# The first batch's gate convolution on TensorE as products with diagonal matrices, and the opening loads and splits in another order

## The chip, the cores and the metric

The kernel runs on one core of one Trainium2 chip. The metric is the device time of one execution in microseconds (us), lower is better. The kernel before takes 1178.61 us, the median of three runs (1178.06 to 1179.55).

## What is computed

Three stages follow each other, for four batches of 576 positions (the reference, cut):

```python
scores = scale * np.matmul(q, k.transpose(0, 1, 3, 2))       # 4 x 8 heads, 576 x 576, 64 dims
kth = np.partition(scores, -32, axis=-1)[..., -32:-31]
attn = softmax(np.where(scores >= kth, scores, -1e9))
x = concat_heads(np.matmul(attn, v))                          # 4 x 576 x 512
gate_pre[:, s, :] = sum(conv_w[k] * xp[:, s + k, :] for k in range(5))   # xp: 4 zero rows, then x
x = sigmoid(gate_pre) * (x @ w_val) @ w_out
u = x + np.real(np.fft.fft(np.fft.fft(x, axis=1), axis=2))
out = u + np.maximum(norm(u) @ w_ch1, 0) @ w_ch2              # 512 -> 2048 -> 512
```

The convolution is per feature: each of the 512 features has its own five taps.

## The kernel before

Every engine has its own list of instructions, written out in one function for each engine (sync for the DMA queue, tensor, scalar, vector, gpsimd), and they meet by semaphores. All five run the same main loop over **slots**, `for s in plan`. A tile is 128 query rows of one head (or the last 64 rows of both heads of a pair); a pair of heads has 9 tiles (`TILES`), a batch 4 pairs, 36 tiles (`NT`). In slot s tile s enters and older tiles move on:

- TensorE, `scores(s)` (L442): fp32r products of the high parts of the queries with high and low parts of the keys. `transpose_p(s-6)` (L455) turns the exponents of tile s-6. `attend(s-7)` (L471, L475) multiplies with v where a unit of the output ends (tiles 1, 3, 5, 7 and 8 of a pair); it needs the reciprocal of the sums.
- ScalarE, in this order: `copy_scores(s)` (L648), `store_pT(s-6)` (L668), `exponent(s-5)` (L655, L660), `split_weights(s-2)` (L686), the step of the second half of the kernel, `store_out(s-7)` (L677), `gate_tanh` (L690), then the high parts for the next pair (`high_queries` L635 to L638, `high_keys` L642).
- VectorE: in odd slots `reciprocal(s-6)` (L801, L803), in even ones `select(s-1, 0)`, then for odd slots the rest of a pair of tiles, `select(s-2, 1)`: four MAX8 (L761, L776) and three MATCH_REPLACE8 (L770) for each tile, two tiles taken in turn, to find the 32nd value of each row. Then the low parts of the second head of the next pair (`split_low`, L790, L792), and `conv` (L816, L819): five taps of 128 x 576 for a channel chunk c of 128 features, one chunk for each pair of heads.
- POOL: `biases(s-5)` (L917, L918; needs the 32nd value), `split_weights(s-2)` (L934), `scale_out(s-7)` (L929, writes x_new, the input of the convolution), low parts of the first head of the next pair (`split_low`, L907, L909).

In slots 2 to 33 the 32 parts of w_ch1 and w_ch2 are split into a high (fp32r) part by ScalarE and the rest by POOL, and written back to DRAM for the later passes. They come through two buffers, u[0] and u[1].

Four feature matrices' products (`feature_weights`, L482) run in slots 6, 8, 10 and 12. From slot 43 on, the steps of the batch before (values L482, the Fourier products, projection, and the two layers of 2048, L574 and L588) are spread over the slots by a table of costs (`STEPS`, `COST`). `values` of batch b wait for all of x_new of the batch; VectorE's step (L866) multiplies them with the gate, for which `m_tanh` must have come.

The convolution's places are a table by slot: chunk 0 of batch 0 in slots 21 to 23, chunk 1 in 28 to 30, chunk 2 in 35 to 37, chunk 3 in 43 and 44; batches 1 to 3 the same, 36 slots later each. The opening stands ahead of the loop: the sync queue loads q and k of pair 0 (head 0 to q_raw and k_raw, head 1 to the tile z), v, the identity, and then 4 MB of tables and weights; `load_qk(1, 0)` comes in slot 0 behind them.

## Time and profile before

| what | value |
|---|---|
| median of three runs | 1178.61 us (1178.06 to 1179.55) |
| the profiled execution's own time | 1173.26 us |
| its span in the trace | 1171.5 us |
| mean granted TensorE clock | 0.948 of full |
| TensorE matmuls busy | 1036.1 us, 88% of the span |
| VectorE busy | 872.8 us, 75% |
| ScalarE busy | 617.6 us, 53% |
| POOL busy | 404.1 us, 34% |
| DMA | 200.37 MB, mean 171 GB/s |

The profile is of one execution; what a number of it says of the median holds up to the 5.35 us between 1173.26 and 1178.61. Busy shares are means over a span of which the first quarter (attention of the first batch) and the rest have different limits, so they have to be read by stretch. An engine's "idle before" names who ended the wait.

### The profile page before, as it was taken

How to read it: one execution, taken by the hardware profiler on the slowest of the kernel's cores; microseconds unless marked ns; L12 is line 12 of the kernel's file. 1: busy time of each engine (PE TensorE's matmuls, PEld its weight loads, DVE VectorE, ACT ScalarE, POOL GpSimd, SP SyncE). 2: the span in 40 equal slices, each digit the busy share in tenths (PEclk: the TensorE clock that was granted, in tenths of full speed). 3: DMA queues.
4: the chain of work that ended last, by engine and by line, in shares of the span. 5: the costliest groups of instructions: out<-in, count | busy, mean ns of one | idle time of the engine just before them, and what ended most of it. 6: DMA issues, size and time to landing. Idle time of an engine off the chain costs nothing.

```text
span 1171.5 us, 19830 instructions
## 1 busy us (share of the span) xinstructions
PE 1036.1 (88%) x6608; PEld 827.8 (71%) x6608; DVE 872.8 (75%) x1900; ACT 617.6 (53%) x1253; POOL 404.1 (34%) x704
## 2 busy tenths in 40 slices
PE   2776675589988999999989999999889999999998
PEld 1445554466667888866578888875678888648887
DVE  3999999998998897897898987897988960320000
ACT  2676675645466665645466756455565654012211
POOL 1443552223344422332443423233443222233221
PEclk9986566789999999999999999999999999999999
DMA  6755456111256675620367675411367555207974
GB/s 199 228 178 174 156 189 231 32 31 57 68 172 227 246 257 208 205 67 21 112 222 253 251 231 199 145 57 59 134 204 259 201 211 196 99 1 288 343 269 164
DMA packets 81188, 200.37 MB, mean 171 GB/s; under 512 B 8384, under 2 KB 26560, under 8 KB 81088
## 3 DMA queue, kind: packets, MB, share of 16 engines
q1 hardware_dynamic: 81088, 199.11, 50.2%
q8 instruction: 54, 0.88, 0.3%
q14 instruction: 46, 0.38, 0.1%
HBM read 177.58 MB, written 21.50 MB: 170 GB/s over the span
## 4 chain that ended last, share of the span: by engine, by line
PE 38%; issue 26%; DVE 18%; POOL 12%; ACT 3%; SPq 1%; DMA 1%; POOLq 0%; DVEq 0%; ACTq 0%
PE p_m L482 11%; PE p_m L588 10%; PE p_m L574 10%; DVE rest L770 8%; DVE top L776 6%; POOL hid_lo L982 3%; PE p_t L455 2%; PE p_t L471 2%; POOL bias L918 2%; PE p_s L442 2%; POOL bias L917 2%; DVE top L761 1%; ACT prob L655 1%; POOL x_new L929 1%; POOL gate L941 1%
## 5 line engine op out<-in xcount | busy, mean ns | idle before, releaser
L776 DVE MAX8 top<-rest 128x8 f32<-128x576 f32 x432 | 304.6, 746 | 0.0
L770 DVE MATCH_REPLACE8 rest<-top,rest 128x576 f32<-128x576 f32 x288 | 211.7, 743 | 0.0
L982 POOL TENSOR_TENSOR hid_lo<-hid,hid_hi 128x256 fp32r<-128x256 f32 (+1 forms) x128 | 105.0, 820 | 302.5 <-ACT hid_hi L717 302.5
L588 PE MATMUL p_m<-w_st,hid_hi 128*128 128x512 f32 x640 | 202.3, 397 | 1.5 <-POOL hid_lo L982 1.5
L574 PE MATMUL p_m<-un_hi,w_st 128*128 128x320 f32 (+1 forms) x1024 | 165.6, 304 | 13.3 <-ACT hid_hi L717 9.5
L655 ACT ACTIVATE prob<-s_sb,bias 128x576 f32<-128x576 f32 x144 | 111.1, 771 | 104.3 <-POOL bias L918 104.0
L574 PEld LDWEIGHTS p_m<-un_hi,w_st 128*128 128x128 f32 x1024 | 142.8, 189 | 26.4 <-issue 23.4
L455 PE MATMUL p_t<-id_sb,prob 128*128 128x128 f32 x720 | 118.3, 299 | 45.1 <-ACT prob L660 23.7
L471 PE MATMUL p_t<-pT,v_sb 128*64 128x128 f32 (+1 forms) x1600 | 111.8, 293 | 38.2 <-issue 26.1
L648 ACT ACTIVATE s_sb<-p_s 128x576 f32<-128x576 f32 x144 | 93.2, 647 | 96.2 <-PE p_s L442 96.0
L442 PE MATMUL p_s<-k_hi,q_st 128*128 128x512 f32 (+1 forms) x320 | 116.1, 365 | 29.7 <-ACT s_sb L648 19.9
L471 PEld LDWEIGHTS p_t<-pT,v_sb 128*64 128x64 f32 x1600 | 92.2, 153 | 67.1 <-issue 50.7
L588 PEld LDWEIGHTS p_m<-w_st,hid_hi 128*128 128x128 f32 x640 | 113.4, 189 | 20.7 <-POOL hid_lo L982 3.0
L588 PE MATMUL p_m<-w_st,hid_lo 128*128 128x512 f32 x320 | 127.0, 397 | 0.0
L716 ACT ACTIVATE hid<-p_m 128x256 f32<-128x256 f32 (+1 forms) x128 | 51.5, 403 | 139.7 <-PE p_m L574 139.7
L660 ACT ACTIVATE prob<-prob,bias 128x576 f32<-128x576 f32 x144 | 111.8, 776 | 13.1 <-ACT prob L655 0.4
L455 PEld LDWEIGHTS p_t<-id_sb,prob 128*128 128x128 f32 x720 | 82.6, 149 | 50.1 <-ACT prob L660 44.4
L761 DVE MAX8 top<-s_sb 128x8 f32<-128x576 f32 x144 | 101.4, 744 | 11.9 <-ACT s_sb L648 11.9
L668 ACT ACTIVATE pT<-p_t 128x640 f32<-128x640 f32 x144 | 101.4, 704 | 14.8 <-PE p_t L455 14.7
L770 DVE MATCH_REPLACE8 rest<-top,s_sb 128x576 f32<-128x576 f32 x144 | 105.7, 741 | 0.0
L442 PEld LDWEIGHTS p_s<-k_hi,q_st 128*128 128x128 f32 x320 | 66.8, 209 | 53.8 <-issue 29.7
L853 DVE TENSOR_TENSOR u<-p_m,u 128x512 f32<-128x512 f32 (+1 forms) x20 | 12.6, 681 | 112.9 <-PE p_m L588 112.9
(83 smaller groups left out, 1580.1 us busy)
## 6 DMA issues: line engine op xcount, KB each, us to landing
w_st<-w_split SPq DMA_DIRECT2D x256, 512.0 KB, 4.5
w_split<-w_st SPq DMA_DIRECT2D x32, 512.0 KB, 3.0
q_raw<-qT SPq DMA_DIRECT2D x62, 144.0 KB, 2.9
k_raw<-kT SPq DMA_DIRECT2D x62, 144.0 KB, 3.0
u<-w_ch SPq DMA_DIRECT2D x32, 256.0 KB, 3.4
v_sb<-v SPq DMA_DIRECT2D x16, 256.0 KB, 3.6
wslot<-w_val SPq DMA_DIRECT2D x4, 1024.0 KB, 5.3
wslot<-w_out SPq DMA_DIRECT2D x4, 1024.0 KB, 5.3
```

Source lines behind the costliest of these rows:

```text
L442: mm = pe.matmul(p_s[:, k0:k1], q_st[h][p % 2][:, cols], k[:, k0:k1], start=n == 0, stop=n == len(parts) - 1)
L455: mm = pe.transpose(p_t[:, c * P:c * P + P], prob[t % 3][:, c * P:c * P + P], id_sb[:, :])
L471: pe.matmul(p_o[D * h:D * h + D, 0, 0:n], v_sb[p % 2][:, c, D * h:D * h + D], pT[tt % 3][:, c, c0:c0 + n], start=c == 0, stop=c == NCH - 1 ...
L482: mm = pe.matmul(bank[0:m, c0:c1], a, w, start=k == 0, stop=k == len(lhs) - 1, skip_group_check=True)
L574: mm = pe.matmul(mbank(HIDDEN_BANK[g], n), w1_st[i % NB1][:, w, k, :], x[:, k, at:at + n], start=part + k == 0, stop=part + k == KC + 1)
L588: mm = pe.matmul(mbank(j), h[i % 2][:, P * j:P * j + P], w2_st[i % NB2][:, w, :], start=f == 0 and part == 0, stop=f == FC - 1 and part == 2)
L655: act.activation(prob[t % 3][:, 0:S], s_sb[t % NS][:, :], ACT.Prelu, bias=bias[t % NK][:, 1:2], scale=-BIG, alpha=1.0 / BIG).then_inc(s_dr ...
L660: act.activation(prob[t % 3][:, 0:S], prob[t % 3][:, 0:S], ACT.Exp, bias=bias[t % NK][:, 0:1], scale=-SCALE, accum_out=psum_row[:, t % NK: ...
L761: dve.max(top[tt % NK][:, 0:8], s_sb[tt % NS][:, :]).then_inc(s_chain, 1)
L770: dve.match_replace(rest[tt % 2][:, :], top[tt % NK][:, 8 * n - 8:8 * n], src[:, :], LOWEST).then_inc(s_chain, 1)
L776: found = dve.max(top[tt % NK][:, 8 * n:8 * n + 8], rest[tt % 2][:, :])
L982: pool.tensor_tensor(hid_lo[i % 2][:, 0:WIDTH[g]], hid[:, 0:WIDTH[g]], hid_hi[i % 2][:, 0:WIDTH[g]].bitcast(F32), ALU.subtract).then_inc(m ...
```

## The change

The convolution of batch 0 alone leaves VectorE. POOL makes, in slots 14 to 17, twenty diagonal matrices of 128 x 128 (identity times one tap of one chunk, `make_diags`), five in a slot, in tiles that are not yet in use. TensorE makes each chunk as two groups of five fp32 products of 288 columns (`convolve`), in slots 16, 25, 34 and 43, between the transposes and the step or attend. ScalarE's tanh of the chunk reads the two PSUM banks, in the same slot, between `store_pT` and `exponent`. The five taps on VectorE of batches 1 to 3 stay.

At the opening the four loads of pair 0's head 0 go out on two queues (keys on sync, queries on ScalarE's), VectorE makes the low keys that POOL made, `load_qk(1, 0)` is issued behind the identity and ahead of the 4 MB, and the high and low parts of pair 1 are made in slots 2 to 6 rather than 0 to 6.

```diff
-HALF = 256
+HALF, HALF_S = 256, S // 2
...
+HIGH_Q0, HIGH_K0, LOW0 = {2: 0, 5: 1}, {3: 0, 5: 1}, {3: 0, 6: 1}
+CONV_BANK = [1, 2]
+DIAG_AT = {14: 0, 15: 1, 16: 2, 17: 3}
+CONV0_AT = {TILES * (c + 1) + ATTEND: c for c in range(KC)}
...
+        def split_at(s, first, others):
+            p, i = divmod(s, TILES)
+            h = (others if p else first).get(i)
+            return (p + 1, h) if h is not None and p + 1 < ALL_PAIRS else None
...
         def conv_due(s):
-            return [(b, c, taps) for b in range(B) for c, taps in CONV_AT.get(s - NT * b, [])]
+            return [(b, c, taps) for b in range(1, B) for c, taps in CONV_AT.get(s - NT * b, [])]
...
+        diags = [ab[:, :], un[0][:, :], un[1][:, :], u[2][:, :], u[3][:, :]]
+        def diag(c, k):
+            n = TAPS * c + k
+            return diags[n // 4][:, P * (n % 4):P * (n % 4) + P]
...
-                load_qk(0, 0)
+                for half in range(2):
+                    sp.dma_start(k_raw[D * half:D * half + D, :], kT[0, 0]).then_inc(s_qk_in[0], 16)
                 load_qk(0, 1)
                 sp.wait_ge(s_zero, FILLS)
                 load_v(0)
                 sp.dma_start(id_sb[:, :], ident).then_inc(s_const, 16)
+                load_qk(1, 0)
                 sp.dma_start(gv[:, :, 0:DM], feat.rearrange("(c q) n -> q c n", q=P)).then_inc(s_setup, 16)
...
                 for s in plan:
                     p, i = divmod(s, TILES)
-                    if s == 0:
-                        load_qk(1, 0)
...
+                def convolve(c):
+                    pe.wait_ge(s_diag, TAPS * (c + 1))
+                    pe.wait_ge(s_x, 5 * (c + 1))
+                    if c:
+                        pe.wait_ge(m_tanh, c)
+                    else:
+                        pe.wait_ge(s_feat_ev, KC)
+                    for o in range(2):
+                        for k in range(TAPS):
+                            mm = pe.matmul(mbank(CONV_BANK[o], HALF_S), diag(c, k),
+                                           x_new[c][:, k + o * HALF_S:k + o * HALF_S + HALF_S], start=k == 0, stop=k == TAPS - 1,
+                                           skip_group_check=True)
+                    mm.then_inc(s_conv, 1)
...
+                    elif j == 2 and b == 0:
+                        pe.wait_ge(m_tanh, KC)
...
                     if s in FEAT_SLOTS:
                         feature_weights(FEAT_SLOTS.index(s))
+                    if s in CONV0_AT:
+                        convolve(CONV0_AT[s])
...
                 def gate_tanh(b, c):
+                    if b:
+                        act.wait_ge(m_conv, TAPS * (KC * (b - 1) + c + 1))
+                        act.activation(gate[:, c, :], gate[:, c, :], ACT.Tanh).then_inc(m_tanh, 1)
+                    else:
+                        act.wait_ge(s_conv, c + 1)
+                        at = BANK * CONV_BANK[0]
+                        act.activation(gate[:, c, :].rearrange("p (o n) -> p o n", o=2),
+                                       p_m[:, at:at + 2 * BANK].rearrange("p (o n) -> p o n", o=2)[:, :, 0:HALF_S],
+                                       ACT.Tanh).then_inc(m_tanh, 1)
...
-                for h in range(2):
-                    high_queries(0, h)
-                    high_keys(0, h)
+                for half in range(2):
+                    act.dma_start(q_raw[D * half:D * half + D, :], qT[0, 0]).then_inc(s_qk_in[0], 16)
+                high_keys(0, 0)
+                high_queries(0, 0)
+                high_queries(0, 1)
+                high_keys(0, 1)
...
                     if due(s, TRANSPOSE):
                         store_pT(s - TRANSPOSE)
+                    if s in CONV0_AT:
+                        gate_tanh(0, CONV0_AT[s])
                     if due(s, EXPONENT):
                         exponent(s - EXPONENT)
...
+                dve.wait_ge(s_hi, 1)
+                dve.tensor_tensor(k_lo[0][0][:, :], k_raw[:, :], k_hi[0][0][:, :].bitcast(F32),
+                                  ALU.subtract).then_inc(s_lo[0], 1)
                 split_low(0)
...
-                    pool.tensor_tensor(k[:, :], k_in, high[:, :].bitcast(F32),
-                                       ALU.subtract).then_inc(s_lo[0], 1)
+                    if p:
+                        pool.tensor_tensor(k[:, :], k_in, high[:, :].bitcast(F32),
+                                           ALU.subtract).then_inc(s_lo[0], 1)
...
+                def make_diags(c):
+                    pool.wait_ge(s_resid, 80)
+                    pool.wait_ge(s_const, 16)
+                    for k in range(TAPS):
+                        pool.tensor_scalar(diag(c, k), id_sb[:, :], cw_sb[:, c, k:k + 1], None, ALU.mult).then_inc(s_diag, 1)
...
                     if part_due(s) is not None:
                         split_weights(part_due(s))
+                    if s in DIAG_AT:
+                        make_diags(DIAG_AT[s])
```

`high_queries`, `high_keys` and both `split_low` are now called through `split_at` with the tables `HIGH_Q0`, `HIGH_K0`, `LOW0` for pair 1 and the old tables for all others. The old `conv` of chunk 0 no longer waits for the feature products.

How the rows move, first on POOL in slots 14, 15 and 16 (bias2, bias3 and bias4 belong to tiles 10 to 12). Before:

```order
L934 TENSOR_TENSOR w1_st0<-u0,w1_st0 128x512 [waits s_whi]
L929 TENSOR_TENSOR x_new0<-or_sb1 128x128 [waits s_or]
L917 TENSOR_SCALAR bias2<-top2 128x1 [waits s_exp,s_topk]
L918 TENSOR_SCALAR bias2<-top2 128x1
L934 TENSOR_TENSOR w1_st1<-u1,w1_st1 128x512 [waits s_whi]
L929 TENSOR_TENSOR x_new0<-or_sb0 128x64 [waits s_or]
L917 TENSOR_SCALAR bias3<-top3 128x1 [waits s_exp,s_topk]
L918 TENSOR_SCALAR bias3<-top3 128x1
L934 TENSOR_TENSOR w1_st2<-u0,w1_st2 128x512 [waits s_whi]
L917 TENSOR_SCALAR bias4<-top4 128x1 [waits s_exp,s_topk]
L918 TENSOR_SCALAR bias4<-top4 128x1
```

After:

```order
L984 TENSOR_TENSOR w1_st0<-u0,w1_st0 128x512 [waits s_whi]
L991 TENSOR_SCALAR ab<-id_sb,cw_sb 128x128 [waits s_const,s_resid]
L991 TENSOR_SCALAR ab<-id_sb,cw_sb 128x128 x3
L991 TENSOR_SCALAR un0<-id_sb,cw_sb 128x128
L979 TENSOR_TENSOR x_new0<-or_sb1 128x128 [waits s_or]
L967 TENSOR_SCALAR bias2<-top2 128x1 [waits s_exp,s_topk]
L968 TENSOR_SCALAR bias2<-top2 128x1
L984 TENSOR_TENSOR w1_st1<-u1,w1_st1 128x512 [waits s_whi]
L991 TENSOR_SCALAR un0<-id_sb,cw_sb 128x128 [waits s_const,s_resid]
L991 TENSOR_SCALAR un0<-id_sb,cw_sb 128x128 x2
L991 TENSOR_SCALAR un1<-id_sb,cw_sb 128x128 x2
L979 TENSOR_TENSOR x_new0<-or_sb0 128x64 [waits s_or]
L967 TENSOR_SCALAR bias3<-top3 128x1 [waits s_exp,s_topk]
L968 TENSOR_SCALAR bias3<-top3 128x1
L984 TENSOR_TENSOR w1_st2<-u0,w1_st2 128x512 [waits s_whi]
L991 TENSOR_SCALAR un1<-id_sb,cw_sb 128x128 [waits s_const,s_resid]
L991 TENSOR_SCALAR un1<-id_sb,cw_sb 128x128
L991 TENSOR_SCALAR u2<-id_sb,cw_sb 128x128 x3
L967 TENSOR_SCALAR bias4<-top4 128x1 [waits s_exp,s_topk]
L968 TENSOR_SCALAR bias4<-top4 128x1
```

Between each slot's weight part and its x_new, or the next slot's bias, there are now five TENSOR_SCALAR.

On TensorE in slot 16 (the products with ab and un0 are convolution 0, p_s is the next tile's scores). Before:

```order
L455 MATMUL p_t<-id_sb,prob1 128x128 [waits s_or,s_pT,s_exp]
L455 MATMUL p_t<-id_sb,prob1 128x128 x4
L442 MATMUL p_s<-k_hi01,q_st01 128x512 [waits s_copy,s_lo1,s_lo0]
L442 MATMUL p_s<-k_lo01,q_st01 128x512
```

After:

```order
L476 MATMUL p_t<-id_sb,prob1 128x128 [waits s_or,s_pT,s_exp]
L476 MATMUL p_t<-id_sb,prob1 128x128 x4
L522 MATMUL p_m<-x_new0,ab 128x288 [waits s_feat_ev,s_x,s_diag]
L522 MATMUL p_m<-x_new0,ab 128x288 x3
L522 MATMUL p_m<-x_new0,un0 128x288
L522 MATMUL p_m<-x_new0,ab 128x288 x4
L522 MATMUL p_m<-x_new0,un0 128x288
L463 MATMUL p_s<-k_hi01,q_st01 128x512 [waits s_copy,s_lo1,s_lo0]
L463 MATMUL p_s<-k_lo01,q_st01 128x512
```

Ten products now stand between the transposes of tile 10 and the scores of tile 17.

On ScalarE in the same slot (s_sb4 is the copy of tile 16, prob2 the exponent of tile 11). Before:

```order
L648 ACTIVATE s_sb4<-p_s 128x576 [waits s_drop,s_qk]
L668 ACTIVATE pT1<-p_t 128x640 [waits s_pv,s_tr]
L655 ACTIVATE prob2<-s_sb5,bias3 128x576 [waits s_tr,s_bias]
L660 ACTIVATE prob2,psum_row<-prob2,bias3 128x576 [waits s_drop,s_radd]
L686 ACTIVATE w1_st2<-u0 128x512 [waits s_w1put2,s_wraw0]
```

After:

```order
L687 ACTIVATE s_sb4<-p_s 128x576 [waits s_drop,s_qk]
L707 ACTIVATE pT1<-p_t 128x640 [waits s_pv,s_tr]
L734 ACTIVATE gate<-p_m 128x576 [waits s_conv]
L694 ACTIVATE prob2<-s_sb5,bias3 128x576 [waits s_tr,s_bias]
L699 ACTIVATE prob2,psum_row<-prob2,bias3 128x576 [waits s_drop,s_radd]
L725 ACTIVATE w1_st2<-u0 128x512 [waits s_w1put2,s_wraw0]
```

The tanh that waits for TensorE's products (s_conv) stands ahead of the exponent.

## Rows read from the trace of the kernel before

**Rows 1.** The page's part 2: busy tenths and granted clock in 40 equal slices.
```profile
DVE  3999999998998897897898987897988960320000
...
PEclk9986566789999999999999999999999999999999
```

**Rows 2.** Stretches: length, PE, PEld, DVE, ACT, POOL busy (count), PEclk, DMA share, GB/s.
```profile
60.00:228.00 168.00, 109.02 (x696) 88.40 (x695) 167.27 (x358) 111.99 (x210) 67.12 (x107) 0.70 0.52 166
84.00:98.00 14.00, 8.84 (x57) 7.36 (x55) 13.96 (x32) 9.98 (x19) 6.00 (x11) 0.74 0.49 150
...
272.00:1171.00 899.00, 862.45 (x5567) 690.96 (x5566) 621.93 (x1344) 451.51 (x945) 307.94 (x545) 0.99 0.51 176
```

**Rows 3.** VectorE in order of time: start, us, line, operation, tiles, count.
```profile
114.54 1.40 DVE L761 MAX8 top<-s_sb 128x8 f32<-128x576 f32 x2
...
220.19 1.41 DVE L761 MAX8 top<-s_sb 128x8 f32<-128x576 f32 x2
...
230.10 1.40 DVE L761 MAX8 top<-s_sb 128x8 f32<-128x576 f32 x2
...
240.00 1.40 DVE L761 MAX8 top<-s_sb 128x8 f32<-128x576 f32 x2
...
244.09 0.80 DVE L790 TENSOR_TENSOR q_st<-q_raw,q_st 64x512 fp32r<-64x512 f32 x2
```

**Rows 4.** POOL in order of time, slots 11 to 15.
```profile
70.38 1.40 POOL L909 TENSOR_TENSOR k_lo<-k_raw,k_hi 128x576 fp32r<-128x576 f32 x1
...
76.58 0.22 POOL L917 TENSOR_SCALAR bias<-top 128x1 f32<-128x1 f32 x1
...
80.92 0.22 POOL L917 TENSOR_SCALAR bias<-top 128x1 f32<-128x1 f32 x1
...
85.15 0.47 POOL L929 TENSOR_TENSOR x_new<-or_sb 128x128 f32<-128x128 f32 x1
85.70 0.22 POOL L917 TENSOR_SCALAR bias<-top 128x1 f32<-128x1 f32 x1
```

**Rows 5.** The opening in order of time, and the DMA issues from 11.5 to 13 us.
```profile
10.35 0.74 DVE L792 TENSOR_TENSOR k_lo<-z,k_hi 128x576 fp32r<-128x576 f32 x1
...
22.47 0.68 ACT L635 ACTIVATE q_st<-q_raw 128x576 fp32r<-128x576 f32 x1 [10.50 <-DMA k_raw<-kT]
...
23.72 0.76 DVE L761 MAX8 top<-s_sb 128x8 f32<-128x576 f32 x1 [10.96 <-ACT s_sb L648]
...
u<-w_ch SPq DMA_DIRECT2D x2, 256.0 KB, 7.6
```

**Rows 6.** All engines in order of time, slots 15 to 19.
```profile
89.92 0.32 POOL L929 TENSOR_TENSOR x_new<-or_sb 128x64 f32<-128x64 f32 x1
...
92.67 0.77 ACT L655 ACTIVATE prob<-s_sb,bias 128x576 f32<-128x576 f32 x1
...
94.21 0.18 ACT L660 ACTIVATION_READ_ACCUMULATOR prob<-prob,bias 128x1 f32 x1
...
98.79 0.15 DVE L801 TENSOR_SCALAR rinv<-psum_row 128x2 f32<-128x2 f32 x1
...
99.23 2.40 PE L471 MATMUL p_t<-pT,v_sb 128*64 128x128 f32 x20 [4.01 <-issue]
...
108.69 0.19 DVE L801 TENSOR_SCALAR rinv<-psum_row 128x2 f32<-128x2 f32 x1
```

**Rows 7.** Lines L819 and L816 alone from 20 to 280: length, DVE busy (count), PEclk, DMA.
```profile
20.00:280.00 260.00, 14.76 (x16) 0.79 0.46 144
...
20.00:280.00 260.00, 2.00 (x4) 0.79 0.46 144
```

**Rows 8.** TensorE in order of time, slots 43 to 45.
```profile
242.21 4.05 PE L482 MATMUL p_m<-x_new,wslot 128*128 128x257 f32 x16
...
249.81 1.31 PE L471 MATMUL p_t<-pT,v_sb 128*64 128x128 f32 x20
...
257.84 1.08 PE L455 MATMUL p_t<-id_sb,prob 128*128 128x128 f32 x5 [3.55 <-ACT or_sb L677]
```

30 lines of the change are left out of this document (12 added, 18 removed).

## The prediction

> **What bounds the kernel now.** I read the slices of the page first, then stretches, then single engines in order of time. A slot is one pass of the main loop: one tile enters, older ones move on.
>
> The slices [rows 1] show three parts. Up to about 25 us nobody is steadily busy. Then VectorE is at 9 up to a quarter of the span, and TensorE's granted clock at 5 to 8 in most of those slices. The stretches say it in numbers [rows 2]: from 60 to 228 VectorE is busy 167.27 of 168 us and TensorE 109; from 272 on TensorE is busy 862.45 of 899. So a microsecond taken from the first 272 us should arrive at the end, and VectorE holds most of those. VectorE's slot costs 4.95 us: pairs of tiles start at 230.10 and 240.00 [rows 3].
>
> But there is a second chain just behind it, **the split loop**. In slots 2 to 33 POOL writes a bias, ScalarE does the tile's exponent and then splits a weight part, POOL subtracts the remainder, and only then comes POOL's next bias. Its steps [rows 4] are 4.34 us (76.58 to 80.92) and, with an x_new piece, 4.78 (80.92 to 85.70). What POOL idles in a step is no slack, since it is ScalarE's part of the chain. Nine slots of the loop cost 4 x 4.34 + 5 x 4.78 plus two subtractions for low halves, 1.40 each [rows 4], together 44.0 us. VectorE's nine slots cost 9 x 4.95 plus its own low halves, 0.80 [rows 3] and 0.74 [rows 5], together 46.1, and with a channel's taps 49.9. Those taps are busy 14.76 + 2.00 us in four channels [rows 7]; less some 0.085 us by which neighbours overlap, twenty times, 3.77 a channel. Taking the convolution off VectorE leaves only 2.1 us in nine slots until the loop is the bound. The two chains meet in VectorE's reciprocal, which waits for the exponent. In slot 17 that exponent ends at 94.39 and the reciprocal starts at 98.79 [rows 6]: slack 4.4 us.
>
> **The opening.** Now the second tile's first MAX8 starts at 23.72 [rows 5], because ScalarE waits till 22.47 for q_raw of pair 1, and the copy of tile 1 stands behind it. In the change the four loads of pair 0 lie on two queues, so the last is issued about 1.2 us earlier (two issues of 0.6), VectorE and POOL make the low halves side by side (1.40 us less [rows 4]), and tile 1's copy has no load ahead of it. Head 1 lands 1.2 us earlier too, so VectorE ends its low halves at about 9.8 where it now ends at 11.09 [rows 5], tile 1 is scored and copied (1.5 + 0.65 us), and the second MAX8 starts at about 12.1: **-11.6 us on VectorE**.
>
> Of this some is given back at once. The first two weight parts are issued between 11.5 and 13 us and take 7.6 us to land, the first at about 19.5 [rows 5]; in the change pair 1's four loads (0.6 each) stand ahead of it: about 22. ScalarE waits for it in slot 2; split, high queries and the copy of tile 3 queued behind (0.6 to 0.7 each) end at 24.0, while VectorE, 11.6 us early, wants that copy at 21.8: +2.2. Head 1 of pair 1 is loaded only after POOL's slot 3, with weight part 3 behind it, and holds ScalarE in slot 5: by the same steps I take +1.0 for VectorE's low halves and +2.7 for two reciprocals after them. Together +5.9. VectorE reaches slot 17 some 5.7 us early, at 93.1, the split loop only 2.5 to 3 us early, as its start hangs on that same landing.
>
> **The diagonals.** 20 TENSOR_SCALAR of 128x128 on POOL, five in each of slots 14 to 17. No row has this form. Below it is a 128x1 TENSOR_SCALAR, 0.22 us; above, a TENSOR_TENSOR of 128x128, 0.47 [rows 4], and I add 0.10 us between two of them, since a TENSOR_SCALAR never starts before the end of the one ahead. One input rather than two puts it nearer the middle: 0.35 + 0.10, so 2.2 us a slot (1.6 to 2.8, which is -2.6 or +2.4 over the four slots). They stand before the slot's x_new and the next bias, inside the loop. The Trainium skill's page "GPSIMD Engine Reference", section "Engine selection", says that one-input elementwise work runs there at roughly line rate and two-input work at half of it; by it the lower half of my bounds would hold, 1.6 to 2.2 a slot. The trace has only the two-input half of that comparison.
>
> **The convolution on TensorE.** Ten fp32 matmuls of 288 columns for each channel. The rate is that of the values: eight instructions (two records each) with 2304 columns in 4.05 us at full clock [rows 8], 1.76 ns a column, so 2880 columns take 5.1 us; at the lower of the two levels, 1.2 GHz against 2.4 (attend takes 2.40 us at 99.23 and 1.31 at 249.81 [rows 6, 8]) 10.1. The granted clock was 0.74 from 84 to 98 [rows 2], so I take 7.3 us in slot 16. ScalarE waits for it in slot 16 **ahead of the exponent of tile 11**, adds a tanh of about 0.7 (a ScalarE pass over 576 columns is 0.68 [rows 5]), then goes on. In time: x_new of tile 8 ends at 90.24 now [rows 6]; -2.5 for the opening, +4.4 for two slots of diagonals gives 92.1; TensorE to 99.4; tanh to 100.2; exponent (92.67 to 94.39, 1.7 [rows 6]) to 101.9. VectorE wants it at 93.1 and starts at 102.0: a stall of 8.9, and now it is **3.2 us later than before** (98.79).
>
> Then slots 16 and 17: split and remainder to 103.9, diagonals 106.1, bias and exponent of tile 12 to 108.5, split and remainder 110.4, diagonals 112.6, x_new, bias, exponent of tile 13 to 115.4. The reciprocal of slot 19 starts at 108.69 now [rows 6], then at 115.5: **+6.8**.
>
> From pair (18,19) to (36,37), 18 slots, VectorE now takes 105.6 us (114.54 to 220.19 [rows 3]) with three channels' taps (11.3). Without them it needs 94.3, but the loop needs 2 x 44.0 and, in slots 25 and 34, a convolution plus tanh of 8.1 each: 104.2. So those 11.3 us bring **-1.5**, which leaves +5.3. After slot 33 there are no splits and VectorE's own 4.95 us a slot hold, unchanged.
>
> **Slot 43.** Convolution 3 stands before the values of batch 0. The clock is high there (attend takes 1.31 at 249.81 [rows 8]): +5.1 us of TensorE at 242.21. In exchange VectorE loses 3.8 us of taps, and TensorE's wait of 3.55 us before 257.84 [rows 8] is filled. TensorE's last work before that wait ended at about 254.3 (257.84 less 3.55); 254.3 + 5.1 against 257.84 is +1.5, less 0.4 for a smaller wait of the same kind near 272. From there TensorE is the bound, and the sum is carried to the end.
>
> Sum: -11.6 + 5.9 (opening), +8.9 and +3.6 (slots 16 to 19), -1.5 (the next 18 slots), +1.1 (slot 43) = **+6.4 us** over the profiled execution of 1173.26, so 1179.7. That execution is 5.35 under the median of the three runs, 1178.61, and the forecast for a median is **1185.0**. Bounds: the diagonals -2.6 or +2.4; three convolutions at full clock -6.6, or at half in slot 16 and one more +5.6. So about 1176 to 1193. A measurement tells from no change about 0.2%, 2.4 us.
>
> **Rivals.**
> *The loop has room (VectorE alone decides).* If POOL and ScalarE fall into place as VectorE hurries, the opening's 11.6 and three channels' 11.3 are kept, and slot 43 costs 1.1: 1178.6 - 21.8 = 1156.8. For it: from 60 to 228 POOL is busy 67 us of 168 and ScalarE 112 [rows 2]. Against: the loop's step of 4.34 is made of durations, and the reciprocal's slack is 4.4 us, not 20. It decides only if the exponent of tile 11 ends before 93. Chance 0.05.
>
> *The added work releases the clock.* Now TensorE falls to the lower level again and again between 60 and 260 us [rows 1]. If convolutions and earlier matmuls hold it at full, each convolution takes 5.1, transposes and attends in the loop shrink, and the diagonals may be at their low bound: 6.4 - 6.6 - 2.6 is -2.8, so 1175.8. Page "TensorE: Matmul & The Clock Gate", section "What's actually happening", in the Trainium skill has the rule that the throttled state is the default and activity releases it. The trace agrees as far as the clock goes up after TensorE had been busy (0.70 where it is busy 109 of 168 us, 0.99 where it is busy 862 of 899 [rows 2]). Against it: outside the convolutions VectorE still sets TensorE's pace, and gaps remain. Chance 0.14.
>
> *Nearly even.* The loop starts 5 rather than 2.5 us early, or the diagonals are cheap while one convolution runs warm: the stalls shrink by 4 to 6, 1179 to 1181. Chance 0.15.
>
> *The loop is hit harder.* TensorE's scores and transposes of slot 17 also wait behind the cold convolution, and slots 25 and 34 stall VectorE by more than I take: two convolutions at 10.1, diagonals at 0.47: 6.4 + 5.6 + 2.4 = 14.4, so 1193.0. Chance 0.16.
>
> **Numbers.** The forecast has 0.50 within 1181 to 1189. Faster by over 0.2% (under 1176.2): the first two rivals, less the part of the second that lies inside, 0.17. Within: the third and a little of the forecast's low end, 0.16. Slower: 0.67.
>
> **What the new profile should show.** The second MAX8 near 12 us. ScalarE idle about 7 us before the first tanh, and VectorE idle 6 to 10 us before a reciprocal near 100, released by ScalarE's exponent; 2 to 4 us more near 112 and 1 to 3 at later reciprocals. POOL's diagonal at 0.3 to 0.47. The pair (40,41), now at 240.00, near 245. The values of batch 0 start about 10 us later than 242.21, of which some 4 are won back by 272. TensorE unchanged from there on. It is wrong if VectorE has no idle before its reciprocals around slot 17, or if that pair starts before 235.

## The result, and the profile after

The changed kernel takes **1183.31 us**, the median of 12 runs (1178.79 to 1184.24); the kernel before takes 1178.14 us, the median of 12 (1174.14 to 1179.55). The ratio is 1.0041, with a 95% interval from 1.0028 to 1.0055: slower by 0.3 to 0.6%. The forecast was 1185.0, slower.

The profiled execution of the changed kernel took 1184.24 us, at the top of its runs; that of the kernel before took 1173.26, below all twelve. So the two traces stand 11.0 us apart, the medians 5.2. That matters below.

The page of the changed kernel: busy time, the granted clock in 40 slices, and the chain of work that ended last.

```profile
PE 1052.0 (89%) x6688; PEld 836.3 (71%) x6688; DVE 861.6 (73%) x1881; ACT 617.9 (52%) x1253; POOL 413.5 (35%) x723
...
PEclk9987587799999999999999999999999999999999
...
PE 43%; issue 27%; POOL 17%; ACT 5%; DVE 4%; DMA 2%; SPq 1%; POOLq 0%; ACTq 0%; DVEq 0%
```

The last of these lines is the chain that ended last, by engine. Before it was:

```profile
PE 38%; issue 26%; DVE 18%; POOL 12%; ACT 3%; SPq 1%; DMA 1%; POOLq 0%; DVEq 0%; ACTq 0%
```

VectorE's share of it falls from 18% to 4%, and POOL's rises from 12% to 17%.

VectorE's busy time fell by 11.2 us (872.8 before): the taps of four channels are 15.1 us less, the low keys that POOL made are 0.8 more, and the TENSOR_SCALAR ahead of the reciprocals took 3.1 more in sum (15.8 against 12.7). Still the kernel is slower. The view by line, from 20 to 300 us, says what took its place (busy, mean ns, then the idle time before these instructions and who ended it):

```profile
L851 DVE TENSOR_SCALAR rinv<-psum_row 128x2 f32<-128x2 f32 x22 | 7.7, 350 | 27.8 <-ACT prob L699 27.8
```

Before, the same reciprocals had 1.2 us of idle in that stretch:

```profile
L801 DVE TENSOR_SCALAR rinv<-psum_row 128x2 f32<-128x2 f32 x22 | 4.6, 210 | 1.2 <-ACT prob L660 1.2
```

Where it is lost shows VectorE in order of time (start, length, engine, line, operation, and in brackets the idle time before it and who ended it), against 98.79, 108.69, 114.54, 220.19 and 240.00 before [rows 3, 6]:

```profile
13.55 0.76 DVE L811 MAX8 top<-s_sb 128x8 f32<-128x576 f32 x1 [1.59 <-ACT s_sb L687]
...
106.69 0.17 DVE L851 TENSOR_SCALAR rinv<-psum_row 128x2 f32<-128x2 f32 x1 [10.15 <-ACT prob L699]
...
121.73 0.17 DVE L851 TENSOR_SCALAR rinv<-psum_row 128x2 f32<-128x2 f32 x1 [5.02 <-ACT prob L699]
...
127.56 1.40 DVE L811 MAX8 top<-s_sb 128x8 f32<-128x576 f32 x2
...
230.04 1.40 DVE L811 MAX8 top<-s_sb 128x8 f32<-128x576 f32 x2
...
249.85 1.40 DVE L811 MAX8 top<-s_sb 128x8 f32<-128x576 f32 x2
...
276.02 1.42 DVE L811 MAX8 top<-s_sb 128x8 f32<-128x576 f32 x2
```

The second MAX8 is 10.2 us earlier than before (23.72 [rows 5]); the reciprocal of slot 17 is 7.9 us later, that of slot 19 13.0 later, the pair (18,19) 13.0, (36,37) 9.9, (40,41) 9.9 and (44,45) 8.3 (267.70 before). At slot 17 VectorE still had 2.3 us of the opening's gain (96.54 against 98.79); two stalls within 25 us, 15.2 us together, cost that and 13 us more.

The chain that makes them, read backwards from 106.69, over POOL, TensorE and ScalarE in order of time:

```profile
93.55 2.96 POOL L991 TENSOR_SCALAR un<-id_sb,cw_sb 128x128 f32<-128x128 f32 x5
96.47 0.32 POOL L979 TENSOR_TENSOR x_new<-or_sb 128x64 f32<-128x64 f32 x1
96.88 0.23 POOL L967 TENSOR_SCALAR bias<-top 128x1 f32<-128x1 f32 x1
97.20 0.30 POOL L968 TENSOR_SCALAR bias<-top 128x1 f32<-128x1 f32 x1
107.27 1.27 POOL L984 TENSOR_TENSOR w_st<-u,w_st 128x512 fp32r<-128x512 f32 x1 [9.76 <-ACT w_st L725]
```
```profile
96.89 4.18 PE L522 MATMUL p_m<-x_new,ab 128*128 128x288 f32 x8 [3.65 <-POOL un L991]
...
103.70 0.65 PE L522 MATMUL p_m<-x_new,un 128*128 128x288 f32 x2
103.97 0.61 PE L463 MATMUL p_s<-k_hi,q_st 128*128 128x512 f32 x1
```
```profile
104.39 0.65 ACT L734 ACTIVATE gate<-p_m 128x576 f32<-128x576 f32 x1 [10.40 <-PE p_m L522]
104.93 0.77 ACT L694 ACTIVATE prob<-s_sb,bias 128x576 f32<-128x576 f32 x1
105.79 0.77 ACT L699 ACTIVATE prob<-prob,bias 128x576 f32<-128x576 f32 x1
```

POOL makes five diagonals ahead of the last piece of x_new, TensorE starts the convolution when that piece is there (96.89) and takes 7.5 us (to 104.35), ScalarE stands 10.40 us before its tanh with the exponent of tile 11 queued behind, though that exponent's bias was ready at 97.5, and POOL stands 9.76 us for the weight part that ScalarE splits after it. The bracket names "un", a diagonal, as what TensorE waited for; the diagonals ended 96.51, x_new 96.79, and the start at 96.89 fits the latter.

### The profile page after: what moved, and what is told of

Its sections match the earlier page's. It is cut to its first block, busy times and chain, and to the rows that moved or that the text cites. A ratio compares the mean times of both kernels' runs of the same rounds, so it can differ in the third digit from the quotient of the medians.

```text
span 1182.4 us, 19988 instructions
## 1 busy us (share of the span) xinstructions
PE 1052.0 (89%) x6688; PEld 836.3 (71%) x6688; DVE 861.6 (73%) x1881; ACT 617.9 (52%) x1253; POOL 413.5 (35%) x723
## 4 chain that ended last, share of the span: by engine, by line
PE 43%; issue 27%; POOL 17%; ACT 5%; DVE 4%; DMA 2%; SPq 1%; POOLq 0%; ACTq 0%; DVEq 0%
PE p_m L503 13%; PE p_m L625 11%; PE p_m L611 10%; POOL hid_lo L1038 3%; PE p_t L492 3%; PE p_t L476 3%; PE p_s L463 2%; POOL bias L968 2%; ACT prob L694 2%; POOL bias L967 2%; POOL w_st L984 2%; POOL q_st L956 1%; POOL k_lo L959 1%; POOL x_new L979 1%; DMA k_raw<-kT 1%
## 5 line engine op out<-in xcount | busy, mean ns | idle before, releaser
L463 PE MATMUL p_s<-k_hi,q_st 128*128 128x512 f32 (+1 forms) x320 | 113.5, 357 | 25.0 <-ACT s_sb L687 15.1
L492 PE MATMUL p_t<-pT,v_sb 128*64 128x128 f32 (+1 forms) x1600 | 107.1, 285 | 20.6 <-ACT pT L707 20.6
L492 PEld LDWEIGHTS p_t<-pT,v_sb 128*64 128x64 f32 x1600 | 87.9, 147 | 49.5 <-ACT pT L707 26.9
L707 ACT ACTIVATE pT<-p_t 128x640 f32<-128x640 f32 x144 | 101.3, 703 | 15.3 <-PE p_t L476 15.2
```

Source lines behind the costliest of these rows:

```text
L463: mm = pe.matmul(p_s[:, k0:k1], q_st[h][p % 2][:, cols], k[:, k0:k1], start=n == 0, stop=n == len(parts) - 1)
L492: pe.matmul(p_o[D * h:D * h + D, 0, 0:n], v_sb[p % 2][:, c, D * h:D * h + D], pT[tt % 3][:, c, c0:c0 + n], start=c == 0, stop=c == NCH - 1 ...
```

## The experiments

The theory: the split loop (POOL's bias, ScalarE's exponent and split, POOL's remainder) has little slack, and the diagonals on POOL and the convolution ahead of the exponent lengthen it. The rivals: the moved opening costs; TensorE's added products cost by themselves; the diagonals alone cost. Each kernel ran beside the kernel before on the same chip; open_only to tanh_late shared one chip, diag_alone to early_late a second, diag_opening and halves a third, open_tanh and halves_old_opening a fourth. Between such groups the ratios to the kernel before are what compares, and the text says so where they tell another size than the medians. A median is of 4 to 12 runs. Starts are of the profiled executions, "18 slots" is from pair (18,19) to pair (36,37).

| kernel | median us | ratio, 95% interval | reciprocal of slot 17 / 19 | pair (18,19) | 18 slots | pair (40,41) |
|---|---|---|---|---|---|---|
| before | 1178.1 | | 98.79 / 108.69 | 114.54 | 105.65 | 240.00 |
| changed | 1183.3 | 1.0041 (1.0028 to 1.0055) | 106.69 / 121.73 | 127.56 | 102.48 | 249.85 |
| open_only | 1171.2 | 0.9941 (0.9929 to 0.9954) | 96.06 / 105.96 | 111.77 | 105.51 | 237.10 |
| conv_only | 1183.6 | 1.0042 (1.0025 to 1.0059) | 106.46 / 121.48 | 127.31 | 101.20 | 248.32 |
| no_diag | 1169.2 | 0.9922 (0.9908 to 0.9936) | 98.96 / 108.88 | 115.58 | 98.66 | 234.05 |
| tanh_late | 1172.1 | 0.9961 (0.9941 to 0.9981) | 97.18 / 114.16 | 119.99 | 98.03 | 238.93 |
| diag_alone | 1178.8 | 1.0009 (0.9999 to 1.0020) | 98.19 / 113.24 | 119.07 | 107.38 | 246.26 |
| one_tap | 1170.2 | 0.9934 (0.9920 to 0.9948) | 101.85 / 116.89 | 122.72 | 95.67 | 240.04 |
| diag_early | 1177.2 | 1.0004 (0.9986 to 1.0022) | 105.35 / 115.28 | 122.01 | 98.70 | 240.52 |
| early_late | 1174.2 | 0.9962 (0.9946 to 0.9979) | 102.83 / 112.72 | 118.55 | 97.92 | 236.99 |
| diag_opening | 1170.2 | 0.9950 (0.9937 to 0.9963) | 96.82 / 106.74 | 113.46 | 101.02 | 234.29 |
| open_tanh | 1166.0 | 0.9890 (0.9864 to 0.9916) | 93.52 / 106.00 | 111.83 | 97.41 | 229.06 |
| halves | 1158.6 | 0.9857 (0.9841 to 0.9873) | 94.91 / 104.81 | 110.63 | 93.12 | 223.56 |
| halves_old_opening | 1163.7 | 0.9878 (0.9858 to 0.9898) | 100.10 / 110.00 | 115.80 | 93.48 | 229.10 |

### The two parts alone

open_only puts batch 0's convolution back on VectorE and makes no diagonals.

```diff
-DIAG_AT = {14: 0, 15: 1, 16: 2, 17: 3}
-CONV0_AT = {TILES * (c + 1) + ATTEND: c for c in range(KC)}
+DIAG_AT = {}
+CONV0_AT = {}
-            return [(b, c, taps) for b in range(1, B) for c, taps in CONV_AT.get(s - NT * b, [])]
+            return [(b, c, taps) for b in range(B) for c, taps in CONV_AT.get(s - NT * b, [])]
```

> The changed kernel with batch 0's convolution back on VectorE (diagonals and the products on TensorE gone); the moved opening alone is left. Theory (the split loop on GpSimd and ScalarE stands just behind VectorE): the second tile's MAX8 starts about 10 us earlier than before, 6 us of it are given back by slot 17, and the loop allows VectorE 2.5 to 4.4 us of lead, so the kernel takes 1174 to 1176 us (2.5 to 4.4 less than the 1178.1 before). Rival A (the opening's move itself costs, for example by the chip's shared queues or by the splits that now collide with slots 2 to 6): 1178 us or more. Rival B (the loop has no part in it): the whole 10 us stay, 1168 us.

Measured 1171.21 us. In the trace the theory's size holds: the second MAX8 at 13.36 (10.4 us early), the reciprocal of slot 17 2.7 early, pair (40,41) 2.9 early, and the span 3.7 shorter. The medians differ by 6.7, so by them the kernel lies 2.8 us under the low end I gave, between the theory and rival B. What a trace of the kernel before shows is one of its fastest runs, so 3.7 is the lower reading and 6.7 the one of the medians. The opening by itself is a gain in either.

conv_only has the changed convolution with the old opening (the four loads of pair 0 on one queue, POOL making both low halves, pair 1's loads in slot 0).

```diff
-HIGH_Q0, HIGH_K0, LOW0 = {2: 0, 5: 1}, {3: 0, 5: 1}, {3: 0, 6: 1}
+HIGH_Q0, HIGH_K0, LOW0 = HIGH_Q, HIGH_K, LOW
```

> The changed kernel with the opening's loads and splits as before; the diagonals and the convolution on TensorE alone. Theory: the loop's slack of 4.4 us in slot 17 is used up by three slots of diagonals (3.0 us each) and by the convolution and tanh ahead of an exponent (about 8); the pair's MAX8 of tiles 18 and 19 starts 10 to 14 us later than before, VectorE saves 11.3 us by slot 43, and the kernel takes 1183 to 1190 us. Rival A (the moved opening is what costs): 1178 us or less. Rival B (nothing but TensorE's 28 us more of products counts, one for one where TensorE is on the path): 1180 to 1183 us.

Measured 1183.58 us, and the pair (18,19) at 127.31, 12.8 later than before. The time alone lies 0.6 us above rival B's range and does not part it from the theory; the late pair, and no_diag below, do. The two kernels with the convolution on TensorE, with the early opening and without, meet in slot 17 within 0.23 us (106.69 and 106.46). In the latter VectorE arrives later and waits less:

```profile
106.46 0.17 DVE L848 TENSOR_SCALAR rinv<-psum_row 128x2 f32<-128x2 f32 x1 [6.24 <-ACT prob L699]
```

That is the plainest sign of a second chain: VectorE comes to it 3.7 us earlier with the early opening (96.54 against 100.22) and waits 3.9 longer. The opening is worth 6.7 us alone, the convolution costs 5.7 alone, and together they are 5.2 slower and not 1.0 faster. Rival A (the opening costs) is gone.

### The links of the loop, one by one

no_diag leaves the diagonals out: the ten products of a chunk take the identity.

```diff
-DIAG_AT = {14: 0, 15: 1, 16: 2, 17: 3}
+DIAG_AT = {}
-                    pe.wait_ge(s_diag, TAPS * (c + 1))
+                    pe.wait_ge(s_const, 16)
-                            mm = pe.matmul(mbank(CONV_BANK[o], HALF_S), diag(c, k),
+                            mm = pe.matmul(mbank(CONV_BANK[o], HALF_S), id_sb[:, :],
```

> The changed kernel without the twenty diagonals: the convolution's ten products of each chunk take the identity as their stationary matrix, at the same places and sizes, so the taps are left out of batch 0's convolution. Theory (the diagonals on GpSimd lengthen the split loop by 3.0 us a slot, 12 in all, in slots 14 to 17): VectorE's wait near 107 shrinks from 10.2 us to 3 or less and the kernel takes 1174 to 1178 us. Rival A (TensorE's added products alone are the cost): 1182 to 1184 us as the changed kernel. Rival B (half and half: the convolution ahead of the exponent would have held the loop up without diagonals too): 1178 to 1181 us.

Measured 1169.22 us, 14 less than the changed kernel by medians and by ratios. TensorE does the same number of products, so rival A of this run (the products alone) is gone. The reciprocal of slot 17:

```profile
98.96 0.17 DVE L851 TENSOR_SCALAR rinv<-psum_row 128x2 f32<-128x2 f32 x1 [1.61 <-ACT prob L699]
```

The wait is 1.61 as expected, and slot 19's reciprocal is 12.85 us earlier than in the changed kernel: four times 2.96 us of diagonals is 11.8, and the convolution took 5.09 us instead of 7.5. Of these 14.2 not all show, since in slot 19 VectorE itself is the later one again.

```profile
91.53 5.09 PE L522 MATMUL p_m<-x_new,id_sb 128*128 128x288 f32 x20 [0.69 <-issue]
```

The kernel came out 5 us better than I expected, since the stalls in slots 25 and 34 shrank too: 18 slots take 98.66 us, not 102.48.

tanh_late moves the four tanh behind exponent and split on ScalarE.

```diff
-                    if s in CONV0_AT:
-                        gate_tanh(0, CONV0_AT[s])
                     if due(s, EXPONENT):
                         exponent(s - EXPONENT)
                     if part_due(s) is not None:
                         split_weights(part_due(s))
+                    if s in CONV0_AT:
+                        gate_tanh(0, CONV0_AT[s])
```

> The changed kernel with batch 0's four tanh moved behind the exponent and the weight part's split on ScalarE, in the same slots. Theory (ScalarE waits 10.4 us for the first convolution with the exponent queued behind it): that wait no longer holds the loop, the four waits for the convolution (27.7 us in sum) fall below 8 us, and the kernel takes 1176 to 1180 us. Rival A (the diagonals alone hold the loop): 1182 to 1184 us. Rival B (TensorE's own time is the cost): 1182 to 1184 us too, with the waits gone.

Measured 1172.06 us, 11.3 less than the changed kernel by medians and 9.4 by ratios, with not one operation fewer, and 4 us under the low end I gave. ScalarE in order of time:

```profile
95.42 0.78 ACT L694 ACTIVATE prob<-s_sb,bias 128x576 f32<-128x576 f32 x1 [3.54 <-POOL bias L968]
96.29 0.77 ACT L699 ACTIVATE prob<-prob,bias 128x576 f32<-128x576 f32 x1
...
102.19 0.65 ACT L734 ACTIVATE gate<-p_m 128x576 f32<-128x576 f32 x1 [4.52 <-PE p_m L522]
```

Tile 11's exponent is 9.5 us earlier (95.42 against 104.93). But the wait for the convolution did not fall below 8 in sum, as I wrote: 13.2 us are left from 20 to 300, and now they hold up the copy of the scores and the next exponent, so slot 19 still stalls 6.46 us. The wait was moved to a better place, not removed.

diag_alone is open_only with the diagonals made in slots 14 to 17 and used by nothing (one line: `DIAG_AT` as in the change).

> The kernel of open_only (1171.2 us) with the twenty diagonals made in slots 14 to 17 and used by nothing: batch 0's convolution stays on VectorE. Theory (12 us more on the split loop, against a slack of 4.4 us less the 2.8 by which VectorE is early there): VectorE stalls 6 to 9 us at the reciprocals of slots 17 and 19, and the kernel takes 1177 to 1180 us. Rival A (only the convolution and tanh ahead of the exponent hold the loop up): 1171 to 1173 us.

Measured 1178.83 us, 7.6 more than open_only by medians and 8.0 by ratios, with VectorE waiting 2.78 and 5.04 us before the reciprocals of slots 17 and 19, 7.8 together. In the traces it is 7.3 us at the pair (18,19) and 9.2 at (40,41); the 1.9 between them stand in no wait (see "The middle" below). Twelve microseconds of work on an engine that is busy for a third of the span cost about eight.

```profile
98.19 0.17 DVE L849 TENSOR_SCALAR rinv<-psum_row 128x2 f32<-128x2 f32 x1 [2.78 <-ACT prob L697]
113.24 0.17 DVE L849 TENSOR_SCALAR rinv<-psum_row 128x2 f32<-128x2 f32 x1 [5.04 <-ACT prob L697]
```

one_tap keeps the diagonals and all waits and does one tap of five.

```diff
-                        for k in range(TAPS):
+                        for k in range(1):
```

> The changed kernel with one tap of the five in each product group: two products a chunk instead of ten, the other four taps left out of batch 0's convolution; diagonals, tanh and all waits as they are. Theory (ScalarE's wait for the convolution is part of the loop): the four chunks are 5.5 us shorter each on TensorE, the first of them in the loop; the wait near 104 shrinks from 10.4 to about 5 us, and the kernel takes 1175 to 1179 us, as diag_alone with its waits or a little less. Rival A (the diagonals alone are the cost): 1181 to 1184 us. Rival B (TensorE's added 28 us count one for one where it is on the path, four fifths of them gone): 1165 us or less.

Measured 1170.22 us, almost 5 under the low end I gave; ScalarE's first wait is 5.18 us. Its slot 19 is 4.8 us earlier than the changed kernel's (116.89), but the rest came later: the 18 slots take 95.67 us, 6.8 less. With the shorter convolutions of slots 25 and 34 the loop keeps up with VectorE, so the saved taps show there. I had priced only the first convolution.

### Where the diagonals can stand

diag_early makes them in slots 2 to 5, with the taps' load moved up behind the identity's.

```diff
-DIAG_AT = {14: 0, 15: 1, 16: 2, 17: 3}
+DIAG_AT = {2: 0, 3: 1, 4: 2, 5: 3}
                 sp.dma_start(id_sb[:, :], ident).then_inc(s_const, 16)
+                sp.dma_start(cw_sb[:, :, :], conv_w).then_inc(s_const, 16)
...
-                sp.dma_start(cw_sb[:, :, :], conv_w).then_inc(s_resid, 16)
```

> The changed kernel with the diagonals made in slots 2 to 5, where GpSimd waits for the first weight parts, the taps' load moved up behind the identity's; convolution and tanh stay. Theory: 12 us leave the loop, as in no_diag (1169.2), less what they now hold up in slots 2 to 5, where VectorE waits for scores anyway: 1169 to 1173 us. Rival A (they hold the loop up just as much there, since it lags VectorE from its start): 1178 to 1184 us.

A miss: 1177.18 us, 4 above the range I gave and 0.8 under rival A's. Here they stand ahead of POOL's low halves of pair 1 and of the first biases, and the loop starts late; in no_diag the first exponent starts at 33.24.

```profile
40.34 0.77 ACT L694 ACTIVATE prob<-s_sb,bias 128x576 f32<-128x576 f32 x1 [8.75 <-POOL bias L968]
```

early_late is diag_early with tanh_late's order.

> diag_early and tanh_late together: nothing that the change adds stands in the split loop in slots 14 to 17. Theory: both costs are gone and VectorE's 11.3 us of taps and 10 us of opening show as far as the loop lets them: 1163 to 1168 us. Rival A (the loop is bound elsewhere once the worst is gone, each mend alone takes all there is): 1168 to 1171 us, as no_diag. Rival B (the convolution on TensorE costs its own time too): 1171 us or more.

Another miss, for the same reason: 1174.16 us. That is no better than tanh_late alone (0.9962 against 0.9961): what slots 14 to 17 no longer pay, slots 2 to 5 do. Its rival B (TensorE's own time) gave the same number for another cause, and this run does not part the two. open_tanh below does: it differs from this kernel in the diagonals' place alone and is 8.5 us better by the ratios; the undivided convolutions have a price too, a smaller one.

diag_opening makes all of them before POOL's first weight part; the taps' load stays moved up as in diag_early.

```diff
-DIAG_AT = {14: 0, 15: 1, 16: 2, 17: 3}
+DIAG_AT = {0: [0, 1], 1: [2, 3]}
```

> The changed kernel with the diagonals made in slots 0 and 1, in front of the first weight part, where GpSimd waits 15.6 us (8.9 to 24.5) for that part to land; diag_early had made them behind it (25.6 to 49), and there the first bias, and with it the first exponent, came 7.1 us later (40.34 against 33.24). Theory: 12 us of diagonals fit into the 15.6, the first exponent is back near 33, and the kernel is no_diag with its taps: 1168 to 1171 us. Rival A (the place does not matter, the products want the taps' load so early that the first transfers suffer): 1175 us or more.

Measured 1170.22 us. POOL in order of time:

```profile
9.55 3.27 POOL L990 TENSOR_SCALAR ab<-id_sb,cw_sb 128x128 f32<-128x128 f32 x4 [0.84 <-DMA cw_sb<-conv_w]
12.79 4.66 POOL L990 TENSOR_SCALAR un<-id_sb,cw_sb 128x128 f32<-128x128 f32 x8
17.43 4.66 POOL L990 TENSOR_SCALAR u<-id_sb,cw_sb 128x128 f32<-128x128 f32 x8
23.55 1.27 POOL L984 TENSOR_TENSOR w_st<-u,w_st 128x512 fp32r<-128x512 f32 x1 [1.46 <-ACT w_st L725]
```

They end at 22.1, and 1.46 us later the first weight part is ready, no later than in the changed kernel (24.40). So they cost little in this stretch, in which POOL waits for something from outside the loop. Against no_diag, which has none, the kernel is 1.0 us slower by the medians and 3.3 by the ratios, and the pair (40,41) starts 0.2 later. The same operations some three slots later were 6.4 us dearer by ratios.

### Both mended, and a version that beats both kernels

open_tanh is diag_opening with tanh_late's order.

> diag_opening with tanh_late's order on ScalarE, the convolutions whole and in the change's slots: the step between diag_opening (1170.2) and halves (1158.6). Theory (what the loop feels of the convolution is ScalarE's wait for it): 1161 to 1166 us. Rival A (what it feels is TensorE's undivided 5 to 7 us ahead of scores, transposes and the attention's products, wherever the tanh stands): 1167 to 1171 us.

Measured 1165.98 us, at the top of what I gave. Its runs lie far apart (1158.55 to 1168.58), so it does not tell the theory from rival A sharply. Against diag_opening, which differs in the tanh's place alone, it is 4.2 us better by the medians and 7.1 by the ratios; halves is another 7.3 or 3.9 better. The reciprocal of slot 19 still waits 2.12 us.

halves also cuts the convolution of the first three channels into two pieces of five products, in the next two slots, with the tanh a slot later.

```diff
-CONV0_AT = {TILES * (c + 1) + ATTEND: c for c in range(KC)}
+CONV0_AT = {TILES * (c + 1) + ATTEND + 1 + o: [(c, o)] for c in range(KC - 1) for o in range(2)}
+CONV0_AT[TILES * KC + ATTEND] = [(KC - 1, 0), (KC - 1, 1)]
+TANH0_AT = {TILES * (c + 1) + ATTEND + (3 if c < KC - 1 else 0): c for c in range(KC)}
```

> diag_opening with each of the first three chunks' convolution cut into its two halves of five products, in the two slots after (one and two slots later than in the change), and the tanh one slot later still and behind exponent and split on ScalarE; the last chunk stays in slot 43 with its tanh behind exponent and split. Theory: neither ScalarE nor GpSimd has anything more in the split loop, and TensorE's piece per slot is 2.5 us instead of 5.1, so the opening's gain and VectorE's 11.3 us of taps stay: 1160 to 1166 us, the pair of tiles 40 and 41 at 228 to 232 against 240.0 before. Rival A (the loop has no more to give, or the half pieces hold up transposes as the whole did): 1168 us or more.

Measured **1158.64 us**, 0.9857 of the kernel before (0.9841 to 0.9873), 1.4% faster than before and by the ratios 1.8% faster than the changed kernel, with that kernel's own operations. It is better than I gave. Pieces, slots and the tanh's place changed together from open_tanh to halves, so what each is worth was not tried. ScalarE waits 2.5 us for convolutions in all, VectorE 3.8 for exponents:

```profile
L736 ACT ACTIVATE gate<-p_m 128x576 f32<-128x576 f32 x4 | 2.5, 633 | 2.5 <-PE p_m L523 2.5
```
```profile
L853 DVE TENSOR_SCALAR rinv<-psum_row 128x2 f32<-128x2 f32 x23 | 5.9, 257 | 3.8 <-ACT prob L701 3.8
```
```profile
110.63 1.40 DVE L813 MAX8 top<-s_sb 128x8 f32<-128x576 f32 x2
...
203.75 1.41 DVE L813 MAX8 top<-s_sb 128x8 f32<-128x576 f32 x2
...
223.56 1.40 DVE L813 MAX8 top<-s_sb 128x8 f32<-128x576 f32 x2
```

Its 18 slots take 93.12 us, 12.5 less than before: three channels' taps (11.3) and a little more. VectorE alone is the bound there now.

halves_old_opening is halves with conv_only's opening.

> halves with the opening's loads and splits as before the change. Theory (with a free loop the opening's gain is kept, where conv_only and the changed kernel showed none of it): 6 to 9 us more than halves, 1165 to 1168 us. Rival A (the opening's gain is small whatever stands behind it): less than 3 us more than halves, below 1162 us.

Measured 1163.73 us, 1.3 us under the range I gave: 5.1 more than halves by medians and 5.5 at pair (40,41) (229.10 against 223.56), but on another chip, and by the ratios only 2.5 (0.9878 against 0.9857, their intervals overlap). So the opening keeps 2.5 to 5.5 us once the loop is free: less than my 6 to 9, and whether more than the rival's 3 this pair does not settle. In slot 19 it was worth nothing in the changed kernel (121.73 against conv_only's 121.48) and is worth 5.2 here (104.81 against 110.00).

## Why the prediction was right, and where it was right by luck

The mechanism was right: two chains that meet in the reciprocal, and an edit that relieves the one and loads the other. The sum was not as good as 1185.0 against 1183.3 looks. By its own steps, all in the profiled executions:

| step | forecast | measured |
|---|---|---|
| second MAX8 | -11.6 us | -10.2 (13.55) |
| VectorE wants the reciprocal of slot 17 at | 93.1 | 96.5 |
| the split loop is early by | 2.5 | 0 |
| diagonals, per slot | 2.2 | 2.96 to 2.98 |
| x_new of tile 8 ends | 92.1 | 96.8 |
| first convolution | 7.3 | 7.5 |
| stall in slot 17 | 8.9 | 10.15 |
| reciprocal of slot 17 against before | +3.2 | +7.9 |
| reciprocal of slot 19 against before | +6.8 | +13.0 |
| the next 18 slots | -1.5 | -3.2 |
| slot 43 | +1.1 | -1.5 (9.85 to 8.3) |
| from there to the end | 0 | +2.6 |
| sum | +6.4 | +10.9 |

**The opening.** The second MAX8 came at 13.55, not 12.1. The second queue brought nothing: I took 1.2 us off the landing of both heads, but ScalarE's first piece of head 0 starts at 5.66 (5.58 before) and head 1's queries at 8.42 (8.17 before). What was gained is that tile 1's copy no longer stands behind the load of pair 1. Then VectorE gave back 7.9 us by slot 17, where I had 5.9.

**The loop's early start did not exist.** I let the loop start 2.5 us early because its start hangs on the first weight part, and took that lead to slot 17. Tile 0's exponent is 3.4 us earlier (33.17 against 36.59), tile 4's and tile 9's are where they were. Of the kernel before and of the changed one, the first pass of the exponents of tiles 4 and 9:

```profile
56.09 0.77 ACT L655 ACTIVATE prob<-s_sb,bias 128x576 f32<-128x576 f32 x1
...
81.57 0.78 ACT L655 ACTIVATE prob<-s_sb,bias 128x576 f32<-128x576 f32 x1 [0.30 <-POOL bias L918]
```
```profile
56.18 0.77 ACT L694 ACTIVATE prob<-s_sb,bias 128x576 f32<-128x576 f32 x1
...
81.66 0.78 ACT L694 ACTIVATE prob<-s_sb,bias 128x576 f32<-128x576 f32 x1 [0.31 <-POOL bias L968]
```

That step cost me 2.5 us at slot 17. No run tried what swallows the lead, but the traces show where it goes. Tile 1's exponent has nothing left of it (40.80 against 40.87), since in slot 5 ScalarE now waits for a weight part from DRAM, which it did not before (its split started at 38.16):

```profile
37.20 0.63 ACT L725 ACTIVATE w_st<-u 128x512 fp32r<-128x512 f32 x1 [2.36 <-DMA u<-w_ch]
```

Tile 3's exponent is 1.6 us earlier again (49.35 against 50.97) and tile 4's is not: ScalarE waits 1.18 us for the feature product of slot 8, which takes 4.98 us (granted clock 0.69 from 48 to 52) and took 3.60 before (1.00). In halves (1.00) it also takes 3.60 and tile 4's exponent comes at 54.65, in open_tanh (1.00) at 53.23, and in no_diag (0.52) at 57.01. So the second loss goes with the granted clock of the single execution, which no step of my sum had.

**The diagonals** took 0.60 to 0.65 us each, outside my bounds of 0.22 to 0.47, and start some 0.59 apart (the gap of 0.10 that I added is not there), where I had 0.45: 3.0 us a slot. Of the 4.7 us by which slot 17's reciprocal is later than I had it, 2.5 are the loop's lead and 1.5 these; the rest is POOL's subtraction at 91.73, which takes 1.84 us where it took 1.28 before, while VectorE makes its low halves (90.96 to 92.44). Of slot 19's further 1.5 all are the diagonals. My upper bound was the 128x128 TENSOR_TENSOR with two inputs, on the thought that one input cannot be dearer. It can: this POOL row beats that bound by 30%. The Trainium skill's page "GPSIMD Engine Reference", section "Engine selection", calls one-input work on this engine roughly line-rate and has it about two times slower than VectorE for two-input work. In this trace the form with one input is the dearer one, 0.6 against 0.47 us for the same 128 elements, and the measurement decides. A diagonal also reads a per-partition scalar; whether that or the form is what costs was not tried.

**The middle.** For the 18 slots I had taken the greater of VectorE's need (105.6 less 11.3, 94.3) and the loop's (two times 44.0, plus two convolutions with tanh). This rule is borne out by the runs to 1.4 us, once each gets its own convolution: no_diag and diag_early, 5.09 and 0.65 us twice, give 99.5, measured 98.66 and 98.70; diag_opening gives 101.2, measured 101.02; one_tap falls under VectorE's 94.3, measured 95.67; halves has nothing of it in the loop and takes 93.12. In the changed kernel, with convolutions of 6.75 and 5.1 us, it gives 101.2, measured 102.48. So only 3.2 of VectorE's 11.3 us arrive: its waits before the reciprocals of these slots, 1.81, 3.94, 0.15 and 1.32, are most of the rest.

What the rule lacks is that some instructions of POOL and VectorE take longer where they overlap, without a wait in the trace. VectorE's TENSOR_SCALAR ahead of a reciprocal mostly takes 0.14 to 0.17 us; three times in these slots (once before) it takes 1.06 to 1.23, each time while POOL subtracts a weight part:

```profile
200.44 1.29 POOL L984 TENSOR_TENSOR w_st<-u,w_st 128x512 fp32r<-128x512 f32 x1 [2.37 <-ACT w_st L725]
200.69 1.06 DVE L851 TENSOR_SCALAR rinv<-psum_row 128x2 f32<-128x2 f32 x1
```

In diag_alone VectorE has no wait in these 18 slots and they are still 1.7 us longer than before (107.38 against 105.65): these TENSOR_SCALAR take 4.7 us in sum there and 2.6 before. So added work can also shift two engines against each other; this is a matter of 1 to 3 us here, not of the main cost.

**Slot 43** was better than forecast, since a convolution at full clock (5.02 us at 252.24) and a channel's taps fewer on VectorE nearly even out.

**From the profile to the median** I added 5.35 us, the distance of the profiled execution of before to its median. That distance is of one execution and did not carry over: the changed kernel's profiled execution lies 0.9 above its median. The steps were 4.5 us too low in sum, and this offset more than made up for it. That the forecast lies 1.7 us from the measurement is this luck. The forecast by medians was +6.4 and the measurement +5.2; the forecast by traces was +6.4 and the measurement +11.0. How a run of this kernel gets to 1174 or to 1180 stays open.

**The rivals.** "The loop has room" is out by the 10.15 us stall. "The added work releases the clock": the granted clock from 60 to 228 us did rise, from 0.70 to 0.77 (in halves to 0.84), but it was 0.64 from 96 to 104, where the first convolution ran, and with the products at full clock (no_diag, 5.09 us) 2.4 us of the stall would go, not ten. "Nearly even" wanted a lead of 5 us or cheap diagonals, and got neither. "Hit harder" (+14.4) was a little closer to the trace's +11.0 than the forecast's +6.4. The expected values of the new profile: idle before the reciprocal near 100 of 6 to 10 us, found 10.15 at 106.69; idle of some 7 us before the first tanh, found 10.40; 2 to 4 us near 112, found 5.02 at 121.73; the values of batch 0 about 10 us later, found 14.9 (257.10); the pair (40,41) near 245, found 249.85. All point the right way and all were put too low, as the sum of the steps was.

## What to carry to other kernels

When work is moved off the engine that is busy all the time, look for the chain that stands just behind it and price every added step on that chain, whichever engine it runs on and however idle this engine looks: here 12 us on POOL, busy for a third of the span, cost about 8. A wait put ahead of another chain's step on the same engine holds that step up: tile 11's exponent came 9.5 us earlier once the wait of 10.4 us stood behind it. With the same work in smaller pieces and later slots little of the waits was left (2.5 us on ScalarE, 3.8 on VectorE), and 2.5 to 5.5 us of the earlier opening, which could not be seen in the changed kernel, came out as well. And add a profiled execution's distance to its median only as an uncertainty, never as a term.
